# The last stores of a fused attention and mixture-of-experts kernel: an earlier signal, an earlier register read, one wait fewer

## The chip, the cores and the metric

The kernel runs on one core of a Trainium2 chip. A core has TensorE (PE in the profile), VectorE (DVE), ScalarE (ACT), GpSimd (POOL) and SyncE (SP), each with an instruction queue of its own, and 16 DMA engines. The metric is the device time of one execution in microseconds (us), the median over executions. The kernel before takes 640.18 us (median of 3: 639.88, 640.18, 641.45).

## The reference, cut to what matters

Three stages, all in float32, on 1152 tokens with 512 features:

```python
# 1. attention, 2 batches x 8 heads x 576 x 64, only the 32 largest scores of each row are kept
scores = q @ k.T / 8
mask = scores >= (32nd largest of the row)
attn = softmax(where(mask, scores, -1e9)); x = attn @ v
# 2. gated feed-forward: 512 -> 1536 -> 512
xn = x / sqrt(mean(x * x) + 1e-6) * rms_g
x = (silu(xn @ w_gate) * (xn @ w_val)) @ w_out
# 3. mixture of experts: 8 experts, each token goes to the one with the largest logit
e = argmax(x @ router, axis=1); gate = its softmax weight
slot = number of earlier tokens of that expert          # dropped if slot >= capacity = 288
out[token] = gate * (relu(x[token] @ w1[e]) @ w2[e])    # rows of dropped tokens are 0
```

## The kernel before, in words

Attention and the feed-forward run interleaved over 9 tiles of 128 tokens. At the end of each tile GpSimd scatters the token rows, each with its gate weight and its token number, to a DRAM tensor `dispatched_rows` ordered by expert. The change touches nothing there.

The last stage, the one at issue, is a chain over the experts 0 to 7. For each expert the kernel takes the first `MAIN` = 168 of its slots, as two halves (`j` = 0 and 1) of `SLOT` = 84 rows. SP loads the rows and the expert's weights, two experts ahead. For expert `e`:

- PE turns the rows (L842), multiplies by `w1` (`hidden`, L855) and by `w2` (`outputs`, L869) into a result that lies with features on partitions, and turns it back into rows (`turn_back`, L880): four transposes for half 0 into PSUM bank 6, then four for half 1 into bank 7. After the eighth it adds to the semaphore `y_done`.
- ACT scales half 0 by the gate weight (`rows_back` in the scalar block, L1234) and signals `y_act`; DVE does the same for half 1 (L1398) and signals `y_vec`. Both wait for `y_done`.
- GpSimd stores each half by an indirect DMA to the token's row of the output (`store`, L1588): first half 0, when `y_act` allows it, then half 1, when `y_vec` does. Each store adds 16 to its semaphore `stored[j][par]`, where `par` is the expert's parity.

`turn_back` of an expert stands behind `hidden` of the next one, so it is hidden there. For expert 7 nothing follows: its turn, scaling and stores are the end of the program.

If an expert has more than 168 tokens, the rest is done in a second pass. Whether that is so stands in the tile `most`, written by DVE beside expert 0 (L1384, semaphore `most_set`). PE, ACT, GpSimd and SP each read it into a register (`value_load`: L899, L1250, L1594, L410) and branch over the second pass. With this input no expert has so many.

At the end both GpSimd (L1606) and SP (L408) wait for all four `stored` semaphores; SP does so before it reads the count. Then the program's block closes (L94 in the trace): each engine executes a DRAIN, and all meet. In the trace PE, DVE, ACT and SP add to a semaphore with their DRAIN, GpSimd waits for these after its own, and then lets all go.

The order of each engine's instructions is as written in the code; no scheduler moves anything. Around the change the waits alone decide when something runs.

Of the kernel before, what the change touches and what calls it, by code (L numbers as in the profile page):

```python
# [61 lines left out]
def build(nc, q, k, v, w_gate, w_val, w_out, rms_g, r_gate, w1, w2, out, capacity):  # L62
    B, H, S, D = q.shape
    DM, FF = w_gate.shape
    E, _, F = w1.shape
    N = B * S
    NT = N // P
# [26 lines left out]
    with ctx:  # L94
# [3 lines left out]
        def sem(name):  # L98
            return ctx.enter_context(nc.semaphore(name))
# [47 lines left out]
        most = dest[:, 2:4]  # L147
# [44 lines left out]
        def gate_of(e, j):  # L192

            return meta[:, e, j, 0:1] if isinstance(e, int) else meta[:, bass.ds(e, 1), j, 0:1].rearrange("p a w -> p (a w)")
# [22 lines left out]
            "first_spots chosen out_full out_copied picked ranked_set lneg_set spot_base lexp_set gate_step row_ready seen_set dispatched last_dispatched most_set "  # L217

            "meta_in xs_in0 xs_in1 w1_a w1_b w2_a w2_b xt_done xt_act xt_vec h_done h_act h_vec "
            "yt_done yt_act yt_vec y_done y_act y_vec stored00 stored01 stored10 stored11 "  # L220

            "o_w o_x o_xt o_xtc o_h o_hc o_yt o_ytc o_y o_yc o_st o_free").split()
        s = {n: sem(n) for n in names}
# [8 lines left out]
        stored = [[s[f"stored{j}{par}"] for par in range(2)] for j in range(2)]  # L232
# [79 lines left out]
        def _(sp):  # L312
# [64 lines left out]
            def slots_in(e, par):  # L377
                sp.dma_start(xs[par], disp[bass.ds(e * CAP, MAIN), :].rearrange("(j p) w -> p j w", p=SLOT)).then_inc(xs_in[par], 16)
# [16 lines left out]
            def refill(e, par):  # L395

                sp.wait_ge(s["h_done"], e * 4 - 4)
                sp.dma_start(w1_s[par], w1[bass.ds(e, 1)].rearrange("a (c p) f -> p (a c) f", p=P)).then_inc(w1_in[par], 16)
                sp.wait_ge(s["yt_done"], e * 2 - 2)
                sp.dma_start(w2_s[par], w2[bass.ds(e, 1)].rearrange("a (c p) d -> p (a c) d", p=P)).then_inc(w2_in[par], 16)  # L400
                slots_in(e, par)

            with sp.Fori(1, E // 2) as i:
                refill(i * 2, 0)
                refill(i * 2 + 1, 1)
            for j in range(2):
                for par in range(2):
                    sp.wait_ge(stored[j][par], 8 * E)  # L408
            sp.wait_ge(s["most_set"], 1)
            over = sp.value_load(most[0:1, 0:1], min_val=0, max_val=N)  # L410
            with sp.If(over > MAIN):
                with sp.Fori(0, E) as e:

# [8 lines left out]
        def _(pe):  # L422
# [145 lines left out]
            def ffn_out(t, i):  # L568

                _, c0, c1 = OUT[i]  # L570
                for c in range(c0, c1):
                    if c % 4 == 0 or c == c0:
                        pe.wait_ge(s["t_free"], use[f"h{c // 4}", t] + 1)
                    last = mm(blk[0], hid[:, c * P:(c + 1) * P], wo_s[:, c, :], start=(c == 0), stop=(c == CF - 1))  # L574
                if i == len(OUT) - 1:
                    last.then_inc(s["out_full"], 1)
# [296 lines left out]
            def turn_back(e):  # L873
                pe.wait_ge(s["yt_act"], e + 2)
                pe.wait_ge(s["yt_vec"], e + 2)
                pe.wait_ge(s["y_act"], e + 1)
                pe.wait_ge(s["y_vec"], e + 1)
                for j in range(2):
                    for c in range(CD):
                        last = tr(ps[0:SLOT, 6 + j, c * P:(c + 1) * P], yT[:, c, j * SLOT:(j + 1) * SLOT], ident[:])  # L880
                last.then_inc(s["y_done"], 1)

# [4 lines left out]
            with pe.Fori(0, E // 2 - 1) as i:  # L888
                for par in (1, 0):
                    e = i * 2 + (1 if par else 2)  # L890
                    hidden(e, par)
                    turn_back(e - 1)
                    outputs(e, par)
            hidden(E - 1, 1)
            turn_back(E - 2)
            outputs(E - 1, 1, ahead=False)
            turn_back(E - 1)

            over = pe.value_load(most[0:1, 0:1], min_val=0, max_val=N)  # L899
            with pe.If(over > MAIN):  # L900
                with pe.Fori(0, E) as e:
                    pe.wait_ge(s["o_x"], e * 16 + 16)
                    pe.wait_ge(s["o_w"], e * 32 + 32)
                    for c in range(CD):
                        last = tr(ps[:, 0, c * REST:(c + 1) * REST], xs_all[0][0:REST, 0, c * P:(c + 1) * P], ident[0:REST, 0:REST])
                    last.then_inc(s["o_xt"], 1)
                    pe.wait_ge(s["o_xtc"], e + 1)
                    for f in range(C1):
                        for c in range(CD):
                            last = mm(ps[:, 2 + f // 4, (f % 4) * REST:(f % 4 + 1) * REST], w1_s[0][:, c, f * P:(f + 1) * P],  # L910
                                      xT[0][:, c, 0:REST], start=(c == 0), stop=(c == CD - 1))
                    last.then_inc(s["o_h"], 1)
                    pe.wait_ge(s["o_hc"], e + 1)
                    for d in range(CD):
                        for f in range(C1):
                            last = mm(ps[:, 4, d * REST:(d + 1) * REST], w2_s[0][:, f, d * P:(d + 1) * P],
                                      hT[:, f, 0:REST], start=(f == 0), stop=(f == C1 - 1))
                    last.then_inc(s["o_yt"], 1)
                    pe.wait_ge(s["o_ytc"], e + 1)
                    for c in range(CD):  # L920
                        last = tr(ps[0:REST, 6, c * P:(c + 1) * P], yT[:, c, 0:REST], ident[:])
# [4 lines left out]
        def _(act):  # L926
# [39 lines left out]
            def split_weights(m):  # L966

                raw, hi, _, half, cols = split_piece(m)
                act.wait_ge(s[("wg_in", "wv_in")[m // 2 % 2] + str(m // 4)], 16)
                for c in half:  # L970
                    copy(hi[:, c, cols], raw[:, c, cols]).then_inc(s["w_hi_set"], 1)
# [243 lines left out]
            def expert(e, par, back, ahead, later=True):  # L1215
                for n in (0, 2):
                    act.wait_ge(s["h_done"], e * 4 + n + 1)
                    nc.scalar.activation(hT[:, 2 * n:2 * n + 2, :], ps[:, 2, 0:2 * MAIN].rearrange("p (c n) -> p c n", c=2),
                                         ACT.Relu).then_inc(s["h_act"], 1)
                if back:  # L1220
                    rows_back(e - 1, 1 - par, later)
                act.wait_ge(s["yt_done"], e * 2 + 1)
                copy(yT[:, 0:2, :], ps[:, 4, 0:2 * MAIN].rearrange("p (c n) -> p c n", c=2)).then_inc(s["yt_act"], 1)
                if ahead:
                    slots(e + 1, 1 - par)

            def rows_back(e, par, later=True):
                act.wait_ge(s["y_done"], e + 1)

                if isinstance(e, int) and e == 0:  # L1230
                    act.wait_ge(s["meta_in"], 32)
                if later:
                    act.wait_ge(stored[0][par], (e - par) * 8)
                nc.scalar.activation(ys[par][:, 0, :], ps[0:SLOT, 6, :], ACT.Copy, scale=gate_of(e, 0)).then_inc(s["y_act"], 1)  # L1234
# [8 lines left out]
            with act.Fori(1, E // 2 - 1) as i:  # L1243
                expert(i * 2 + 1, 1, True, True)
                expert(i * 2 + 2, 0, True, True)
            expert(E - 1, 1, True, False)
            rows_back(E - 1, 1)

            act.wait_ge(s["most_set"], 1)
            over = act.value_load(most[0:1, 0:1], min_val=0, max_val=N)  # L1250
# [178 lines left out]
        def _(pool):  # L1429
# [164 lines left out]
            over = pool.value_load(most[0:1, 0:1], min_val=0, max_val=N)  # L1594
            with pool.If(over > MAIN):
                pool.sem_inc(s["o_free"], 1)
                for e in range(E):
# [3 lines left out]
                                          ys_all[0][0:REST, 0, :], None, bounds_check=N - 1, oob_is_err=False).then_inc(s["o_st"], 16)  # L1601
                    pool.wait_ge(s["o_st"], 16 * (e + 1))
                    pool.sem_inc(s["o_free"], 1)
            for j in range(2):
                for par in range(2):
                    pool.wait_ge(stored[j][par], 8 * E)  # L1606

# [18 lines left out]
```

## Time and profile before

| | |
|---|---|
| Median of 3 executions | 640.18 us (639.88 to 641.45) |
| The profiled execution's own time | 640.57 us |
| Its span, first to last instruction of the program | 638.8 us |
| Time around the span | 1.8 us |
| PE busy | 611.8 us, 96% of the span |
| DVE / ACT / POOL busy | 411.5 / 328.6 / 265.3 us |
| From the last expert's first transpose back (629.45 us) to the end of the span | 9.3 us |

The span is the time from the first to the last instruction of the program; in the profiled execution 1.8 us lie around it. A DMA's row tells how long the engine needs to issue it, and the data moves afterwards. At the very end nearly all engines show as idle, so shares of busy time say nothing; what is read there are the start times of the sequencers' instructions.

### The profile page before, as it was taken

Reading aid. Unit: us, or ns where it says so; the run is one execution under the profiler, and the core shown is the slowest. Engines: PE = TensorE matmul, PEld = TensorE weight load, DVE = VectorE, ACT = ScalarE, POOL = GpSimd, SP = SyncE. Lnnn points to the kernel's source line nnn. Section 1 sums busy time; section 2 is a strip of 40 time slices with the busy share of each in tenths; the row PEclk is TensorE's granted clock in tenths of the full one; section 3 lists DMA queues with packets and bytes.
Section 4 is the critical chain, followed back from the end, with each engine's and each line's share of the span. In section 5 each row is a group of like instructions: output and inputs, shape, how many; then the busy total and the mean of one; then the engine's idle time right before and its main releaser. Section 6 shows DMA issues by size and latency. Waiting matters only on the chain.

```text
span 638.8 us, 11148 instructions
## 1 busy us (share of the span) xinstructions
PE 611.8 (96%) x3935; PEld 470.0 (74%) x3935; DVE 411.5 (64%) x912; ACT 328.6 (51%) x713; POOL 265.3 (42%) x375
## 2 busy tenths in 40 slices
PE   7799989999999999999999999999999999999994
PEld 5466765875766766766766757757589999999994
DVE  5999999899898997998998998902011111011110
ACT  4777877766767766767756757653110110111100
POOL 1866875464365464553654555542310110011101
PEclk9899999999999999999999999999999999999998
DMA  9999800000000000000000000000696776766501
GB/s 239 214 360 337 244 14 0 16 20 2 17 18 1 18 18 2 16 18 2 18 18 2 1 18 2 9 9 1 211 384 185 263 270 208 279 216 235 174 2 39
DMA packets 55182, 65.45 MB, mean 102 GB/s; under 512 B 32282, under 2 KB 32282, under 8 KB 55132
## 3 DMA queue, kind: packets, MB, share of 16 engines
q1 hardware_dynamic: 53388, 60.05, 29.5%
q0 software_dynamic: 1744, 4.76, 2.0%
q8 instruction: 28, 0.46, 0.3%
q14 instruction: 22, 0.18, 0.1%
HBM read 52.89 MB, written 12.30 MB: 102 GB/s over the span
## 4 chain that ended last, share of the span: by engine, by line
PE 91%; ACT 3%; POOL 2%; issue 1%; DMA 1%; SPq 1%; DVE 0%; POOLq 0%; ACTq 0%
PE ps L574 14%; PE ps L869 12%; PE ps L855 11%; PE ps L526 7%; PE ps L533 7%; PE ps L527 7%; PE ps L507 7%; PE ps L480 6%; PE ps L491 6%; PE ps L465 4%; PE ps L589 2%; DMA w_loads<-in_moe_w_gate 1%; PE ps L702 1%; PE ps L880 1%; ACT pt L928 1%
## 5 line engine op out<-in xcount | busy, mean ns | idle before, releaser
L1563 POOL TENSOR_TENSOR s_ring<-s_ring,z_pair 128x576 f32<-128x576 f32 x72 | 100.7, 1420 | 68.9 <-ACT z_pair L1063 68.9
L1374 DVE MATCH_REPLACE8 w_top<-m,w_top 128x576 f32<-128x576 f32 x144 | 105.7, 741 | 0.0
L1368 DVE MAX8 m<-w_top 128x8 f32<-128x576 f32 x144 | 101.5, 745 | 0.0
L574 PE MATMUL ps<-wo_space,hid 128*128 128x512 f32 x216 | 100.7, 593 | 0.8 <-issue 0.8
L526 PE MATMUL ps<-w_parts,x_hi 128*128 128x512 f32 x196 | 81.7, 417 | 0.0
L527 PE MATMUL ps<-w_parts,x_hi 128*128 128x512 f32 x196 | 77.5, 395 | 0.0
L869 PE MATMUL ps<-arena,w_loads 128*128 128x168 f32 x512 | 75.8, 307 | 0.6 <-issue 0.6
L1588 POOL DMA_INDIRECT out_rows<-arena,s_ring x16 | 15.1, 941 | 147.0 <-DVE arena L1398 144.5
L855 PE MATMUL ps<-arena,w_loads 128*128 128x168 f32 x512 | 74.3, 306 | 0.6 <-ACT arena L928 0.6
L855 PEld LDWEIGHTS ps<-arena,w_loads 128*128 128x128 f32 x512 | 73.3, 190 | 0.9 <-ACT arena L928 0.9
L869 PEld LDWEIGHTS ps<-arena,w_loads 128*128 128x128 f32 x512 | 73.2, 190 | 0.8 <-issue 0.8
L1073 ACT ACTIVATE s_ring<-s_ring,nbias 128x576 f32<-128x576 f32 x72 | 55.5, 771 | 24.2 <-POOL s_ring L1563 24.1
L574 PEld LDWEIGHTS ps<-wo_space,hid 128*128 128x128 f32 x216 | 37.1, 190 | 31.2 <-issue 31.2
L1063 ACT ACTIVATE z_pair<-s_ring,nbias 128x576 f32<-128x576 f32 x72 | 51.7, 769 | 11.0 <-POOL nbias L1551 11.0
L928 ACT ACTIVATE pt<-ps 128x512 f32<-128x512 f32 (+1 forms) x108 | 48.8, 488 | 15.8 <-PE ps L491 15.8
L533 PE MATMUL ps<-w_parts,x_lo 128*128 128x512 f32 x196 | 56.8, 405 | 0.0
L1361 DVE MATCH_REPLACE8 w_top<-m,s_ring 128x576 f32<-128x576 f32 x72 | 53.2, 742 | 0.0
L1355 DVE MAX8 m<-s_ring 128x8 f32<-128x576 f32 x72 | 50.7, 744 | 3.3 <-ACT s_ring L928 3.1
L507 PE MATMUL ps<-pt,arena 128*64 128x128 f32 (+1 forms) x800 | 48.6, 271 | 4.2 <-ACT pt L928 4.2
L507 PEld LDWEIGHTS ps<-pt,arena 128*64 128x64 f32 x800 | 40.2, 139 | 15.8 <-issue 11.0
L1378 DVE MAX8 m<-w_top 128x8 f32<-128x576 f32 x72 | 50.8, 746 | 0.0
L928 ACT ACTIVATE s_ring<-ps 128x576 f32<-128x576 f32 x72 | 45.5, 647 | 9.6 <-PE ps L480 9.6
(143 smaller groups left out, 877.8 us busy)
## 6 DMA issues: line engine op xcount, KB each, us to landing
w_loads<-in_moe_w SPq DMA_DIRECT2D x16, 2048.0 KB, 8.9
dispatched_rows<-drow SPq DMA_DIRECT2D x18, 260.0 KB, 7.1
w_loads<-in_moe_w_gate SPq DMA_DIRECT2D x3, 1024.0 KB, 7.7
w_loads<-in_moe_w_val SPq DMA_DIRECT2D x3, 1024.0 KB, 9.9
wo_space<-in_moe_w_out SPq DMA_DIRECT2D x1, 3072.0 KB, 11.5
arena<-dispatched_rows SPq DMA_DIRECT2D x8, 341.2 KB
out_rows<-drow SPq DMA_DIRECT2D x9, 256.0 KB, 5.2
q_space<-in_q SPq DMA_DIRECT2D x8, 256.0 KB, 3.3
```

The costliest lines, as they stand in the source:

```text
L507: last = mm(oT_ps[a * D:(a + 1) * D, r0:r1], vs[b][:, j, 2 * hp + a, :], pt[:, at + r0:at + r1], start=(j == 0), stop=(j == KC - 1))
L526: mm(bank, x_hi[:, c * P:(c + 1) * P], w_hi[:, c, :], start=(c == 0), stop=False)
L527: mm(bank, x_hi[:, c * P:(c + 1) * P], w_lo[:, c, :], start=False, stop=False)
L533: last = mm(bank, x_lo[:, c * P:(c + 1) * P], w_hi[:, c, :], start=False, stop=(c == CD - 1))
L574: last = mm(blk[0], hid[:, c * P:(c + 1) * P], wo_s[:, c, :], start=(c == 0), stop=(c == CF - 1))
L855: last = mm(ps[:, 2 + n % 2, (f % 2) * MAIN:(f % 2 + 1) * MAIN], w1_s[par][:, c, f * P:(f + 1) * P], xT[par][:, c, :], start=(c == 0), sto ...
L869: last = mm(ps[:, 4 + n, (d % 2) * MAIN:(d % 2 + 1) * MAIN], w2_s[par][:, f, d * P:(d + 1) * P], hT[:, f, :], start=(f == 0), stop=(f == C ...
L928: return nc.scalar.activation(dst, src, ACT.Copy)
L1073: nc.scalar.activation(row, row, ACT.Exp, bias=nbias[:, 2 * (g % 2) + a:2 * (g % 2) + a + 1], accum_out=den[:, t % 2, h:h + 1]).then_inc(s ...
L1368: vec.max(m8[:, 2 * (n % 2) + a, i, :], w_top[:, a, :]).then_inc(s["top_step"], 1)
L1374: vec.match_replace(w_top[:, a, :], m8[:, 2 * (n % 2) + a, i, :], w_top[:, a, :], NEG).then_inc(s["top_step"], 1)
L1563: gp.tensor_tensor(row, row, z_pair[:, a, :], ALU.subtract).then_inc(s["lowered"], 1)
```

## The change

Three edits, all at the end of the program. `turn_back` adds to a new semaphore `y_half` after the fourth of the last expert's eight transposes, and ACT's last scaling waits for that in place of `y_done`. SP reads the overflow count before it waits for the stores rather than after. GpSimd no longer waits for the stores at its end.

```diff
-            "yt_done yt_act yt_vec y_done y_act y_vec stored00 stored01 stored10 stored11 "
+            "yt_done yt_act yt_vec y_half y_done y_act y_vec stored00 stored01 stored10 stored11 "
@@ SP
+            sp.wait_ge(s["most_set"], 1)
+            over = sp.value_load(most[0:1, 0:1], min_val=0, max_val=N)
+
             for j in range(2):
                 for par in range(2):
                     sp.wait_ge(stored[j][par], 8 * E)
-            sp.wait_ge(s["most_set"], 1)
-            over = sp.value_load(most[0:1, 0:1], min_val=0, max_val=N)
             with sp.If(over > MAIN):
@@ PE, turn_back
                     for c in range(CD):
                         last = tr(ps[0:SLOT, 6 + j, c * P:(c + 1) * P], yT[:, c, j * SLOT:(j + 1) * SLOT], ident[:])
+                    if j == 0 and isinstance(e, int) and e == E - 1:
+                        last.then_inc(s["y_half"], 1)
                 last.then_inc(s["y_done"], 1)
@@ ACT, rows_back
-                act.wait_ge(s["y_done"], e + 1)
+                if isinstance(e, int) and e == E - 1:
+                    act.wait_ge(s["y_half"], 1)
+                else:
+                    act.wait_ge(s["y_done"], e + 1)
@@ GpSimd, end of the block
-            for j in range(2):
-                for par in range(2):
-                    pool.wait_ge(stored[j][par], 8 * E)
```

The instructions of SP behind its last refill, in the kernel before. TENSOR_LOAD and the two ISA are the read of the count, COMPARE_AND_BRANCH is the jump over the second pass:

```order
L403 COMPARE_AND_BRANCH
L410 TENSOR_LOAD dest [waits stored11,stored10,most_set,stored01,stored00]
L410 ISA x2
L411 COMPARE_AND_BRANCH
```

and in the changed kernel:

```order
L403 COMPARE_AND_BRANCH
L407 TENSOR_LOAD dest [waits most_set]
L407 ISA x2
L412 COMPARE_AND_BRANCH [waits stored10,stored11,stored01,stored00]
```

The same three instructions now stand ahead of the wait, and only the branch is left behind it.

GpSimd's end in the kernel before, from the last store's issue over the count's read and the second pass (jumped over) to the block's end at L94:

```order
L1588 DMA out_rows<-arena,s_ring 1152x512 [waits y_vec,out_zero]
L1594 TENSOR_LOAD dest [waits most_set]
L1594 ISA x2
L1595 COMPARE_AND_BRANCH
L1600 DMA out_rows<-arena 1152x512 [waits o_yc,out_zero]
L1600 DMA out_rows<-arena 1152x512 [waits o_st,o_yc,out_zero] x7
L1595 UNCONDITIONAL_BRANCH [waits o_st]
L94 UNCONDITIONAL_BRANCH [waits stored10,stored11,stored01,stored00]
```

and in the changed kernel:

```order
L1594 DMA out_rows<-arena,s_ring 1152x512 [waits y_vec,out_zero]
L1600 TENSOR_LOAD dest [waits most_set]
L1600 ISA x2
L1601 COMPARE_AND_BRANCH
L1606 DMA out_rows<-arena 1152x512 [waits o_yc,out_zero]
L1606 DMA out_rows<-arena 1152x512 [waits o_st,o_yc,out_zero] x7
L1601 UNCONDITIONAL_BRANCH [waits o_st]
```

The wait at the end is gone and everything ahead of it stands as before.

## Rows read from the trace of the kernel before

**Rows 1.** Chain that ended last, from 619 us: start, duration (us), what.

```profile
618.91 0.76 PE ps L880 x7
619.67 9.13 PE ps L869 x64
...
629.45 1.06 PE ps L880 x8
630.51 0.02 issue
630.53 0.69 ACT arena L1234
631.23 0.02 issue
631.25 0.02 POOLq L1587
...
631.34 0.55 issue
631.89 0.02 POOLq L1587
...
632.12 0.92 POOL out_rows L1588
...
633.36 0.04 POOLq L1595
```

**Rows 2.** Timelines of ACT, DVE and POOL, from 628 us: start, duration, group, [idle before].

```profile
630.53 0.68 ACT L1234 ACTIVATE arena<-ps,s_ring 84x512 f32<-84x512 f32 x1 [5.80 <-PE ps L880]
...
630.53 0.75 DVE L1398 TENSOR_SCALAR arena<-ps,s_ring 84x512 f32<-84x512 f32 x1 [1.19 <-PE ps L880]
...
632.12 0.94 POOL L1588 DMA_INDIRECT out_rows<-arena,s_ring  x1 [8.65 <-DVE arena L1398]
633.36 0.93 POOL L1588 DMA_INDIRECT out_rows<-arena,s_ring  x1 [0.30 <-issue]
```

**Rows 3.** DMA issues, 631.5 to 640 us: count, median us from issue to landing.

```profile
out_rows<-arena,s_ring POOLq DMA_INDIRECT x2, 2.8
```

**Rows 4.** SP's queue, waits: us in total, times, longest.

```profile
SPq L408 <- DMA out_rows<-arena,s_ring: 45.0, 1, 45.0
```

**Rows 5.** Line L408, L410 and L411: count, duration min/median/max (ns), first and last start (us).

```profile
L408 SPq EVENT_SEMAPHORE  x1: 28/28/28, 636.2 to 636.2; - x1
...
L410 SPq TENSOR_LOAD <-dest x1: 484/484/484, 636.3 to 636.3; - x1
L410 SPq FUSED_REGOPS  x1: 183/183/183, 636.8 to 636.8; - x1
L410 SPq SEQ_ASSERT  x1: 26/26/26, 637.1 to 637.1; - x1
...
L411 SPq COMPARE_BRANCH  x1: 50/50/50, 637.2 to 637.2; - x1
```

**Rows 6.** Line L94, the block's end, columns as before.

```profile
L94 POOLq EVENT_SEMAPHORE  x2: 17/17/17, 638.6 to 638.7; - x2
...
L94 ACTq DRAIN  x1: 8/8/8, 631.5 to 631.5; - x1
...
L94 POOLq DRAIN  x1: 2122/2122/2122, 636.4 to 636.4; - x1
L94 SPq DRAIN  x1: 13/13/13, 637.3 to 637.3; - x1
```

**Rows 7.** Lines L1606 and L880: GpSimd's last waits, PE's turn back.

```profile
L1606 POOLq EVENT_SEMAPHORE  x2: 17/30/43, 633.5 to 636.2; - x2
...
L880 PE MATMUL ps<-ident,arena x64: 272/273/279, 500.2 to 630.2; 128*84 128x128 f32 x64
```

**Rows 8.** Line L1615, the block at the program's start.

```profile
L1615 POOLq DRAIN  x1: 174/174/174, 0.3 to 0.3; - x1
```

**Rows 9.** Lines L1384, L1588 and L900: writing the count; landing; PE's branch.

```profile
L1384 DVE CAST dest<-rt x1: 154/154/154, 481.2 to 481.2; 128x1 int32<-128x1 f32 x1
...
DMA to landing us min/median/max: 2.7/5.1/6.7
...
L900 PEldq COMPARE_BRANCH  x1: 348/348/348, 630.4 to 630.4; - x1
```

## The prediction

> **What bounds the kernel now.** The shares of the page (PE 96%) say that PE sets the time up to its last matmul, and the change takes nothing from there. So I read the end alone, in this order: the chain of waits from 619 us, the timelines of ACT, DVE and POOL, the time to landing, and then, line by line, the sequencers' instructions behind the last store. [rows 1] shows PE's eight transposes from 629.45, ACT's scaling right behind at 630.53, GpSimd released at 631.25, its first store issued at 632.12 and the second at 633.36 [rows 2]. A store lands 2.8 us after its issue [rows 3], so the second has landed at 633.36 + 2.8 = 636.2, and there SP's wait of 45.0 us ends [rows 4, 5]. The chain as printed stops at the second issue; what fills 636.2 to 638.8 must be read from the block's end. There two arrivals compete: SP reads the count and comes to its DRAIN at 637.3 [rows 5, 6]; GpSimd comes to its DRAIN at 636.4, and that takes 2.122 us, to 638.5 [rows 6]. The others have long arrived (ACT at 631.5). So GpSimd's DRAIN ends last, and between its end at 636.4 + 2.12 = 638.55 and the end at 638.8 lies about 0.23 us of meeting. The reader is to see that SP's arrival has 638.55 - 637.34 = 1.2 us to spare.
>
> **Part 1, the half signalled alone.** Eight transposes take 1.04 to 1.06 us [rows 1], one lasts 0.273 [rows 7], so they start (1.04 - 0.27) / 7 = 0.11 us apart, and the fourth ends 4 x 0.11 = 0.44 us ahead of the eighth. ACT has been idle for 5.8 us until then [rows 2], and its other wait, for the store of expert 5, is long over. Its scaling starts at 630.09 and signals at 630.79. GpSimd's first wait ends 0.44 earlier, its sequencer comes to the second wait at 631.89 - 0.44 = 631.45, and DVE, whose start is unchanged, ends at 630.53 + 0.75 = 631.28 [rows 2]: just in time, with 0.17 us left. Two issues stand 633.36 - 632.12 = 1.24 us apart whatever DVE does. So the second store is issued at 632.92 and lands at 636.16 - 0.44 = 635.72. The added signal sits on a transpose that is issued anyway. Bounds: 0 if ACT can't use it, and 0.44 + 0.17 = 0.61 us at most, where DVE becomes what GpSimd waits for. I take 0.44.
>
> **Part 2, the count read early.** TENSOR_LOAD 484, FUSED_REGOPS 183 and SEQ_ASSERT 26 ns are 0.69 us, and with four gaps of 0.03 to 0.04 as those in [rows 1] 0.83 us [rows 5]. They move into SP's idle 45.0 us, which begin at 636.2 - 45.0 = 591.2, and the count has been there since 481.2 [rows 9], so they cost nothing there, and nothing is queued behind them but the wait. Behind the wait stay the branch and the DRAIN: SP arrives 0.83 earlier, by itself. Alone this is worth 0, since GpSimd arrives 1.2 us later than SP.
>
> **Part 3, GpSimd's wait dropped.** Its last waits begin at 633.5 [rows 7], right behind the branch at 633.36 [rows 1]; with part 1 its DRAIN can start at 633.1. It must outlast the second issue, 632.92 + 0.93 = 633.85. The trace shows no DRAIN with a store in flight. From below: 0.174 us, that of the start of the program [rows 8], which would end it at 634.0. From above: its 2.12 us counted anew from the landing at 635.72, so to 637.84. Between them: 2.12 us counted from the last issue's end, 633.85 + 2.12 = 635.97. I take the last, because in the profiled run the 2.12 us pass when all stores have landed and the engine has been idle since 634.3 [rows 2, 6]: nothing of this program is left to wait for, so it is work of the DRAIN's own, which can be done beside the stores.
>
> The Trainium skill, page "VectorE: DVE Perf Modes", section "The DRAIN you can't avoid", says that the DRAINs that frame a kernel are about 12 ns and constant on all engines. SP's 13 ns and ACT's 8 ns [rows 6] agree, GpSimd's 2122 ns don't, and the measurement decides. [...]
>
> **The sum.** SP arrives at 637.34 - 0.83 - 0.44 = 636.07, GpSimd at 635.97: SP is now last, by 0.1 us, and the end comes at 636.07 + 0.23 = 636.30. That is 638.78 - 636.30 = 2.48 us less. The parts do not add up one by one: part 3 alone would leave SP last at 637.34 (1.2 us gained), part 2 on top gives 0.8 more, part 1 the last 0.44. The profiled execution took 640.57, which becomes 638.09; it lies 0.39 above the median of the runs, so as a median 640.18 - 2.48 = 637.7 us, 0.39% less.
>
> **Rivals.**
> A. The DRAIN's 2.12 us begin only when the stores have landed. For it: in the one case that the trace has, they did. Against it: in that case GpSimd itself was kept from starting it earlier. GpSimd arrives at 637.84, the end is 638.07, 0.7 us gained: 639.5 us. Nearly the whole gain of parts 2 and 3 would be gone, since SP's earlier arrival is then again of no use.
> B. The DRAIN is partly hidden: part of its steps are done beside the stores and part wait for them, or each goes slower while descriptors and data move. Half of it behind the landing gives 635.72 + 1.06 = 636.78, the end at 637.0, 1.8 us gained: 638.4 us; three quarters give 638.9.
> C. Part 1 doesn't do what it says: ACT does not start before the eighth transpose, or the sequencer's 0.55 us before its next wait [rows 1] do not move along. Then landing stays at 636.16, SP arrives at 636.51, 2.04 us gained: 638.1 us. Against it: ACT starts 0.02 us behind the transposes' end and GpSimd 0.02 us behind ACT's, so each hangs on the one before.
> D. The other side. GpSimd both writes the stores' descriptors and executes the DRAIN, which now begins during the second store. If it holds that store up, the landing is late. The nearest row is the slowest landing of a store, 6.7 us [rows 9] against 2.8; those had weight loads beside them, so it is an upper bound. Landing at 632.92 + 6.7 = 639.6, SP 0.35 us (637.34 - 0.83 - 636.16) and the meeting 0.23 behind it: 640.2, 1.4 us slower, 641.6 us. It decides the sign from a landing time of 2.8 + 2.48 = 5.3 us on. Against it: the second issue's descriptors are written within its 0.93 us, before which the DRAIN can hardly be served.
>
> The Trainium skill, page "Runtime: NRT & Kernel Launch", section "Instruction fetch mechanics", says that a taken branch to code outside the loaded pages must wait until it is fetched. SP's branch is now the only instruction of the kernel's own behind the landing. Its 50 ns [rows 5] show no such wait; the 348 ns of PE's [rows 9] may. By the rule SP would arrive up to 0.3 us later; by the row nothing changes, and I leave it at nothing.
>
> **How the numbers follow.** Forecast 60%, A 15%, B 13%, C 8%, D 4%. About 0.3% or 1.9 us is what a measurement of this kernel can tell from no change. Forecast (2.48) is over it, but by 0.6 us only, and medians of few runs move by some 0.3 us (the fastest of the three runs before lies 0.3 below the median): I count 53 of its 60 as faster. C (2.04) lies on the bound: 4 of 8. B (1.3 to 1.8) 2 of 13, A none. That makes faster 0.59, same 0.37, slower 0.04. The likeliest case's own range is 637.2 to 638.2. To hold 8 in 10 the range must also reach C, B and A: 637.1 to 639.6. The upper end is A's; the lower is the forecast less twice the 0.3 us by which medians move.
>
> **What would show it.** In the changed kernel's trace: ACT's last scaling starts before the eighth transpose ends and some 0.44 us before DVE's; the issues remain 1.24 us apart; SP's TENSOR_LOAD is at about 591 us, and behind its wait at 635.7 only branch and DRAIN (to 636.1); GpSimd's DRAIN starts at about 633.1 and ends by 636.0, and lasts up to 2.9 us, for it includes the second issue. If it ends at 637.8, A is right; in between, B; if the second store lands over 2.8 us after its issue, D is at work. The prediction is wrong if GpSimd still arrives last by more than 0.2 us.

## The result, and the profile after

The changed kernel takes 638.43 us (median of 7 executions, 638.01 to 639.84) against 640.18 (median of 7, 639.63 to 641.47): 1.75 us less, a ratio of 0.9973 with a 95% interval of 0.9962 to 0.9983. The whole interval lies below 1, so the gain is clear of the noise, though at 0.27% it is slightly under the 0.3% that the prediction took as the least that such a measurement can tell. The forecast was 637.7 in a range of 637.1 to 639.6: right way, inside the range, 0.7 us too low.

The profiled execution of the changed kernel took 639.84 us, the slowest of its seven, and its span is 638.0. Compare ends, not spans: the last expert's first transpose starts at 630.45 here and at 629.45 before, and in the executions below it starts anywhere from 628.2 to 630.5, also in two of the same kernel (630.45 here, 628.73 in e11_after); the last section says what goes with it. From that start to the end of the span it takes 7.59 us instead of 9.33. The difference, 1.74 us, is the gain as the two traces show it. Below, "the tail" is this stretch.

The timeline of the changed kernel from 628 us, start, duration, group and [idle before], answers to [rows 1, 2]:

```profile
630.45 1.04 PE L881 MATMUL ps<-ident,arena 128*84 128x128 f32 x8 [0.65 <-issue]
631.09 0.68 ACT L1240 ACTIVATE arena<-ps,s_ring 84x512 f32<-84x512 f32 x1 [5.36 <-PE ps L881]
631.53 0.75 DVE L1404 TENSOR_SCALAR arena<-ps,s_ring 84x512 f32<-84x512 f32 x1 [1.18 <-PE ps L881]
632.68 0.94 POOL L1594 DMA_INDIRECT out_rows<-arena,s_ring  x1 [8.21 <-DVE arena L1404]
633.92 0.94 POOL L1594 DMA_INDIRECT out_rows<-arena,s_ring  x1 [0.30 <-issue]
```

ACT now starts 0.44 us ahead of DVE, while the transposes still run to 631.49; before, both started at 630.53. The two issues are 1.24 us apart as before. The landing takes 2.8 us as in [rows 3].

The lines L407 (the count's read), L411 and L412 of SP, and L94, the block's end, of the changed kernel, with count, duration min/median/max in ns, first and last start in us; they answer to [rows 5, 6]:

```profile
L407 SPq TENSOR_LOAD <-dest x1: 477/477/477, 592.2 to 592.2; - x1
...
L411 SPq EVENT_SEMAPHORE  x2: 17/22/28, 626.3 to 636.7; - x2
...
L412 SPq COMPARE_BRANCH  x1: 50/50/50, 636.8 to 636.8; - x1
...
L94 POOLq EVENT_SEMAPHORE  x2: 17/17/17, 637.8 to 637.9; - x2
...
L94 POOLq DRAIN  x1: 3721/3721/3721, 634.1 to 634.1; - x1
L94 SPq DRAIN  x1: 13/13/13, 637.0 to 637.0; - x1
```

SP reads the count at 592.2, deep in its idle time, its wait ends at 636.7 with the landing, and it is through at 637.0. GpSimd's DRAIN starts at 634.1, beside the second store's issue, and lasts 3.72 us, to 637.8. So it is still GpSimd that arrives last, 1.08 us behind the landing, where it had been 2.39 us.

### The profile page after: what moved, and what is told of

Its sections match the earlier page's. It is cut to its first block, busy times and chain, and to the rows that moved or that the text cites. A ratio compares the mean times of both kernels' runs of the same rounds, so it can differ in the third digit from the quotient of the medians.

```text
span 638.0 us, 11145 instructions
## 1 busy us (share of the span) xinstructions
PE 613.7 (96%) x3935; PEld 471.0 (74%) x3935; DVE 411.4 (64%) x912; ACT 328.7 (52%) x713; POOL 265.9 (42%) x375
## 4 chain that ended last, share of the span: by engine, by line
PE 92%; ACT 3%; POOL 2%; issue 1%; DVE 0%; POOLq 0%; ACTq 0%
PE ps L575 14%; PE ps L870 12%; PE ps L856 11%; PE ps L527 8%; PE ps L534 7%; PE ps L528 7%; PE ps L508 7%; PE ps L481 7%; PE ps L492 6%; PE ps L466 5%; PE ps L590 2%; PE ps L703 1%; PE ps L881 1%; PE ps L559 1%; ACT pt L931 1%
## 5 line engine op out<-in xcount | busy, mean ns | idle before, releaser
L575 PEld LDWEIGHTS ps<-wo_space,hid 128*128 128x128 f32 x216 | 37.1, 190 | 31.2 <-issue 31.2
L1384 DVE MAX8 m<-w_top 128x8 f32<-128x576 f32 x72 | 50.8, 747 | 0.0
```

## The experiments

Each kernel is one of the two with the edit shown. What its trace, of one execution each, says is collected here. "Landing" is the last increment of the stores' semaphores, "DRAIN" the one at the end of the program, "since" how many DMAs GpSimd has issued between the previous DRAIN and this one; all times in us. e3 and e6 to e10 were run once each, so their times say little and their traces are what counts.

| kernel | parts | since | tail | DRAIN lasts | DRAIN ends behind landing | SP arrives behind landing |
|---|---|---|---|---|---|---|
| before | none | 25 | 9.33 | 2.12 | 2.39 | 1.18 |
| e1_half | 1 | 25 | 8.90 | 2.12 | 2.39 | 1.18 |
| e3_half_early | 1, 2 | 25 | 8.89 | 2.12 | 2.39 | 0.28 |
| e2_nowait | 3 | 25 | 8.11 | 3.72 | 1.08 | 1.18 |
| e7_nowait_early | 2, 3 | 25 | 8.03 | 3.73 | 1.08 | 0.28 |
| after | 1, 2, 3 | 25 | 7.59 | 3.72 | 1.08 | 0.28 |
| e11_after (after again) | 1, 2, 3 | 25 | 7.61 | 3.74 | 1.08 | 0.28 |
| e8_drain_first | 1, 2, 3 | 16 | 7.23 | 3.36 | 0.70 | 0.28 |
| e4_drain6 | 1, 2, 3 | 2 | 6.78 | 2.76 | 0.12 | 0.28 |
| e12_drain6 (e4 again) | 1, 2, 3 | 2 | 6.80 | 2.77 | 0.12 | 0.28 |
| e9_drain6_late_read | 1, 3 | 2 | 7.67 | 2.75 | 0.12 | 1.18 |
| e10_before_drain_first | none | 16 | 8.57 | 1.36 | 1.63 | 1.18 |
| e5_before_drain6 | none | 2 | 8.13 | 0.22 | 0.48 | 1.18 |
| e6_drain_all | none | 2 | 8.12 | 0.21 | 0.48 | 1.18 |

The tail repeats well (7.59 and 7.61, 6.78 and 6.80) where whole executions scatter by more than 1 us, so the verdicts on the parts rest on it. In all 14 the second store lands 2.8 us after its issue.

**The parts one by one.** First part 1 alone:

```diff
 # e1_half: the kernel before, with
+                    if j == 0 and isinstance(e, int) and e == E - 1:
+                        last.then_inc(s["y_half"], 1)
...
-                act.wait_ge(s["y_done"], e + 1)
+                if isinstance(e, int) and e == E - 1:
+                    act.wait_ge(s["y_half"], 1)
+                else:
+                    act.wait_ge(s["y_done"], e + 1)
```

> Part 1 alone: the last expert's first half is signalled after four transposes, both other edits undone. All theories: from the start of the last expert's transposes to the end of the span 9.33 us before, so 9.33 - 0.44 = 8.89 here, with GpSimd's DRAIN still 2.1 us long behind the landing. As a median 0.4 us less than before, too little for the timing to tell. If ACT or GpSimd's sequencer can't use the signal, 9.33.

Tail 8.90, so 0.43 less: as expected. Its ratio to before, 0.9988 (0.9979 to 0.9997), agrees with it. The next has part 3 alone:

```diff
 # e2_nowait: the kernel before, without
-            for j in range(2):
-                for par in range(2):
-                    pool.wait_ge(stored[j][par], 8 * E)
```

> Part 3 alone: GpSimd's wait for the stores dropped, both other edits undone. Theory 'partly hidden' (the DRAIN ends 1.1 us behind the landing of the last store, whatever went before): GpSimd arrives at about the same time as SP, which still reads the count behind the landing (1.18 us behind it): from the transposes to the end 9.33 - 1.2 = 8.1 us. Rival 'own work' (2.12 us counted from the end of the last issue): the same 8.1 us, but the DRAIN ends 0.3 us behind the landing and SP is last by 0.9 us. The two differ in where GpSimd's DRAIN ends.

Tail 8.11, ratio 0.9974 (0.9964 to 0.9983). The two theories differed in where the DRAIN ends. These are the rows of L94 and of L408, SP's wait, of this kernel:

```profile
L94 POOLq DRAIN  x1: 3723/3723/3723, 634.0 to 634.0; - x1
L94 SPq DRAIN  x1: 13/13/13, 637.8 to 637.8; - x1
...
L408 SPq EVENT_SEMAPHORE  x1: 28/28/28, 636.7 to 636.7; - x1
```

Landing at 636.64, DRAIN from 634.0 to 637.7: 1.08 us behind the landing, not 0.3. My "own work" theory, on which the forecast stood, falls; "partly hidden" holds. Then the remaining pairs:

```diff
 # e3_half_early: the changed kernel, GpSimd's wait kept
+            for j in range(2):
+                for par in range(2):
+                    pool.wait_ge(stored[j][par], 8 * E)
 # e7_nowait_early: the changed kernel, y_half gone, ACT waiting for y_done again
...
-                    if j == 0 and isinstance(e, int) and e == E - 1:
-                        last.then_inc(s["y_half"], 1)
...
-                if isinstance(e, int) and e == E - 1:
-                    act.wait_ge(s["y_half"], 1)
-                else:
-                    act.wait_ge(s["y_done"], e + 1)
+                act.wait_ge(s["y_done"], e + 1)
```

> Parts 1 and 2 without part 3: GpSimd's wait for the stores stays. All theories: GpSimd's DRAIN of 2.12 us behind the landing sets the end, the early read is worth nothing, and from the transposes to the end it is the 8.9 us of part 1 alone. SP arrives 0.35 us behind the landing.

> Parts 2 and 3 without part 1. GpSimd's DRAIN ends 1.08 us behind the landing as in the changed kernel and is last; SP arrives 0.35 us behind it. From the transposes to the end 7.59 + 0.44 = 8.03 us. That is only 0.1 less than with part 3 alone (8.11), so part 2 is worth 0.1 us in this kernel and not 0.83.

Tails 8.89 and 8.03, as expected. So the early read is worth nothing while GpSimd waits and drains (8.90 to 8.89), and 0.08 us once it drains beside the stores (8.11 to 8.03). Of the three edits it does the least in this kernel. In e3 the timing of the one execution, 641.22 us, lies above before's median though its tail is 0.43 shorter; its last transposes began at 630.54. One execution says nothing on a tenth of a per cent here.

**What the DRAIN does.** In the kernel before nothing is in flight when it starts, and yet it takes 2.12 us; GpSimd's DRAIN at the program's start took 0.17 [rows 8]. One explanation is that it looks at each DMA that GpSimd has issued since its last DRAIN: nine scatters of rows to the experts and sixteen stores. GpSimd idles 8 us before the last expert's stores, so a further DRAIN can be put there:

```diff
 # e4_drain6: the changed kernel; e5_before_drain6: the kernel before; both with
             for e in range(E):
                 store(e, e % 2)
+                if e in (6,):
+                    gp.drain()
```

> The changed kernel with one more DRAIN on GpSimd, behind the stores of expert 6, where it idles 8.6 us. Theory 'list' (a DRAIN looks at each DMA that GpSimd has issued since its last DRAIN: 9 scatters and 16 stores, 2.12 us / 25 = 0.085 us each): the added DRAIN takes those 23 and ends by 628, hidden; the last one has two DMAs and ends 0.1 to 0.3 us behind the last landing, SP is last, from the transposes to the end 6.9 us against 7.59 of the changed kernel, 0.8 us less as a median (637.6). Rival 'fixed' (a DRAIN behind DMAs costs the same however many there are): the last one ends 1.1 us behind the landing as in the changed kernel, 7.6 us, same median, 638.4.

> The kernel before with one more DRAIN on GpSimd, behind the stores of expert 6. GpSimd's wait for the stores stays, so the last DRAIN starts when all has landed. Theory 'list': it lasts about 2 x 0.085 us plus the 0.17 of an idle DRAIN or less, in place of 2.12; SP is last, and from the transposes to the end 9.33 - 1.2 = 8.1 us. Rival 'fixed': 2.1 us and 9.33 as before.

The rows of L94 of e5_before_drain6, and behind them the added DRAIN:

```profile
L94 POOLq DRAIN  x1: 220/220/220, 635.7 to 635.7; - x1
L94 SPq DRAIN  x1: 13/13/13, 636.6 to 636.6; - x1
```

```profile
L1594 POOLq DRAIN  x1: 4534/4534/4534, 620.9 to 620.9; - x1
```

With the same code behind it, the last DRAIN falls from 2122 to 220 ns because another ran 15 us earlier. SP is now last, and the tail is 8.13, though not a line of the change is in. The executions agree: median 639.04 us (10) against 640.20 (30), a ratio of 0.9977 (0.9966 to 0.9988). In e4_drain6:

```profile
L94 POOLq EVENT_SEMAPHORE  x2: 17/17/17, 636.5 to 636.6; - x2
...
L94 POOLq DRAIN  x1: 2761/2761/2761, 633.6 to 633.6; - x1
L94 SPq DRAIN  x1: 13/13/13, 636.5 to 636.5; - x1
```

The DRAIN ends 0.12 behind the landing, SP 0.28 behind it, and the tail is 6.78. "List" holds, "fixed" falls. The median, 638.32 us, did not show the 0.8 us that were expected (637.6); the two kernels are timed side by side further down. The next two tell what is counted, and how much of it the stores can hide:

```diff
 # e8_drain_first: the changed kernel; e10_before_drain_first: the kernel before; both with
+            gp.drain()
             for e in range(E):
                 store(e, e % 2)
```

> The kernel before with one more DRAIN on GpSimd ahead of the first store; the wait for the stores stays, so the last DRAIN finds all landed. It tells whether DMAs are counted or rows. By DMAs (2.122 us for 25, 0.220 for 2: 0.083 each): 0.22 + 14 x 0.083 = 1.38 us for the 16 stores. By rows (9 scatters of 128 rows and 16 stores of 84, 2496 rows in all, 168 in the last two stores, 0.82 ns a row): 1.18 us. If neither, and only a DRAIN near the end shortens it: 2.12.

It lasts 1.36 us against 1.38 by DMAs and 1.18 by rows. By packets (in the trace 80 for a scatter and 64 for a store) it would be 1.28. DMAs fit best:

```profile
L94 POOLq DRAIN  x1: 1363/1363/1363, 636.7 to 636.7; - x1
```

> The changed kernel with one more DRAIN on GpSimd ahead of the first store, so that the last DRAIN has the 16 stores on its list and not the 9 scatters. It starts while the second store is in flight. Theory 'two sweeps' (the list is gone through twice, 0.042 us each time per DMA, and the second time behind the last landing: 1.08 us with 25 DMAs, 0.11 with 2): it ends 0.11 + 14 x 0.042 = 0.70 us behind the landing. Rival 'one slowed sweep' (0.083 us per DMA when idle, 0.14 with a store in flight, so 13 of 25 were done at the landing): 13 of 16 are done, and it ends 0.3 us behind the landing. From the transposes to the end: 7.2 us by the first, 6.8 by the second.

```profile
L94 POOLq DRAIN  x1: 3356/3356/3356, 633.2 to 633.2; - x1
L94 SPq DRAIN  x1: 13/13/13, 636.1 to 636.1; - x1
```

It ends 0.70 us behind the landing at 635.84, as "two sweeps" said to the hundredth; "one slowed sweep" said 0.3 and falls. The tail is 7.23. And a DRAIN after each expert:

```diff
 # e6_drain_all: the kernel before, with
+                if e in (0, 1, 2, 3, 4, 5, 6):
+                    gp.drain()
```

> The kernel before with a DRAIN on GpSimd behind the stores of each of the experts 0 to 6. By the list theory the first (11 DMAs) ends 0.11 + 9 x 0.042 = 0.49 us behind its landing, each later one (2 DMAs) 0.1 us, and the last, with all landed, lasts 0.22 us as with a single added DRAIN. Span as with that one, since GpSimd idles in between. If what a DRAIN costs grows with all DMAs of the program, the later ones end up to 1.1 us behind their landing.

The first added one, with 11 DMAs, ends 0.50 us behind its landing, the other six, with 2 each, 0.12, and the last lasts 0.21:

```profile
L94 POOLq DRAIN  x1: 210/210/210, 637.5 to 637.5; - x1
```

```profile
L1594 POOLq DRAIN  x7: 3627/6207/7509, 504.4 to 622.8; - x7
```

So an added DRAIN is long because it waits for its stores: 6.1 to 7.5 us for the first five, which have weight loads beside them, and 3.6 for the last two, behind the last weight load. GpSimd idles there anyway, and the tail is that of e5_before_drain6 (8.12 and 8.13). Together: with all landed, 2.12, 1.36 and 0.22 us for 25, 16 and 2 DMAs, 0.083 a DMA; with the last in flight, 1.08, 0.70, 0.50 and 0.12 behind the landing for 25, 16, 11 and 2, 0.042 a DMA. The added DRAINs of the other kernels give two more points on the second line: with 9 DMAs (the scatters, e8 and e10) one ended 0.42 us behind the last scatter's landing, with 23 (e4, e5, e9, e12) 0.99. Half of the time per DMA can pass while DMAs fly, half comes behind the last landing.

**Part 2 again, where nothing covers it.**

```diff
 # e9_drain6_late_read: e4_drain6, with SP's read behind its wait as before
-            sp.wait_ge(s["most_set"], 1)
-            over = sp.value_load(most[0:1, 0:1], min_val=0, max_val=N)
-
             for j in range(2):
                 for par in range(2):
                     sp.wait_ge(stored[j][par], 8 * E)
+            sp.wait_ge(s["most_set"], 1)
+            over = sp.value_load(most[0:1, 0:1], min_val=0, max_val=N)
```

> The changed kernel with the added DRAIN behind the stores of expert 6, but with SP reading the count behind its wait, as in the kernel before. With GpSimd's DRAIN short, SP alone sets the end and part 2 is worth its full 0.83 us: from the transposes to the end 6.78 + 0.83 = 7.61 us. Rival: the read is hidden anyway, 6.8 us.

Tail 7.67 against 6.78: the same edit that is worth 0.08 us beside part 3 is worth 0.88 here, 0.05 more than expected. SP's DRAIN comes 0.90 us later behind the landing; the 0.83 left out that SP's wait for `most_set` moves with the read. It stands at L409 of the kernel before, and from it to the read's start it takes 0.07 us:

```profile
L409 SPq EVENT_SEMAPHORE  x1: 28/28/28, 636.2 to 636.2; - x1
```

**A version that beats both.** The changed kernel and the one with the added DRAIN, on one chip:

> The changed kernel itself, on the same chip as the next. From the transposes to the end 7.6 us, 1.7 us less than before as a median (ratio 0.9973).

> The changed kernel with the added DRAIN behind the stores of expert 6, against the changed kernel on the same chip. The list theory: 6.8 us from the transposes to the end, so 0.8 us less than the changed kernel as a median and 2.5 us (0.4%) less than before, ratio 0.9960. Rival: in executions without a profile's detail the DRAIN costs less than the trace says, and both kernels have one median.

Medians 638.84 us (11 executions) and 637.89 (5) against 640.50 for the kernel before; ratios to before 0.9974 (0.9964 to 0.9983) and 0.9962 (0.9948 to 0.9976). In the earlier measurement e4_drain6 had 638.32 and 0.9965 (0.9954 to 0.9976). Both kernels beat the one before. That the added DRAIN beats the changed kernel is shown by the tails, twice 0.81 us shorter; by the times alone the intervals overlap. All executions of both chips together point the same way (638.60 over 18, 638.06 over 13).

## Why the prediction was right, and where it was not

- **What bounds the end.** Right. GpSimd's DRAIN was last, SP had 1.2 us to spare, and from the last arrival to the end it takes 0.21 to 0.24 us in every trace (0.23 by forecast).
- **Part 1**, forecast 0.44: measured 0.43 (before to e1) and 0.44 (e7 to after). DVE ended 0.17 us ahead of the wait that needs it, as forecast. Rival C falls.
- **Part 2**, forecast to bring SP forward by 0.83, alone worth 0: SP came 0.90 earlier (1.18 to 0.28 behind the landing), for the wait at L409 went with the read. It was not run quite alone; beside part 1, with GpSimd's wait kept, it was worth 0.01. In the sum it was given 0.8; it brought 0.08, because GpSimd stayed last.
- **Part 3**, the step that failed: "it is work of the DRAIN's own, which can be done beside the stores". The DRAIN's time does go with what GpSimd has issued, but only half of it can pass there. Forecast was a DRAIN from 633.85 + 2.12 = 635.97, which is 0.25 behind the landing; it ended 1.08 behind. By the sign that the prediction set for itself, "GpSimd still arrives last by more than 0.2 us", its mechanism was wrong: GpSimd is last by 0.80 us (1.08 - 0.28). Alone the part was worth 1.22 us, as forecast (1.2), but that was luck of the pair: SP was 1.18 behind the landing there, and so covered the DRAIN's 1.08.
- **The sum**, 2.48 forecast and 1.74 measured in the tail: the last arrival was forecast 0.35 us behind the landing (SP) and came 1.08 behind it (GpSimd), which is 0.73 of the 0.74. The added DRAIN takes GpSimd out of the way, and its tail of 6.78 us is close to what the forecast had for the changed kernel (9.33 - 2.48 = 6.85). The median, 638.43, missed the likeliest case's own range (637.2 to 638.2); it lies in the stated one because that was drawn wide enough to reach B and A.
- **Rivals.** It was B. "Half of it behind the landing" (1.06 us, 638.4 us) met both the trace (1.08) and the median (638.43), and had 13%. A asked for 2.12 behind the landing. D did not show: the landing took 2.8 us in every kernel. Nor did the wait for instructions that was weighed for SP's branch: it took 50 ns before and after. The 12 ns by the Trainium skill's page "VectorE: DVE Perf Modes", section "The DRAIN you can't avoid", which it gives for the DRAINs of the runtime's own preamble and postamble, are near those of SP (13 ns) and ACT (8 ns) at the block's end. They do not hold there for DVE, whose DRAIN starts beside its last scaling and takes 786 ns, or for GpSimd after DMAs: 0.21 to 3.74 us, by what it has issued and what is in flight.

The evidence was at hand for a better weighing. A DRAIN of 0.17 us without DMAs and 2.12 with 25 suggested that its time hangs on DMAs. What hangs on a DMA may need that DMA to be over, so B deserved more than 13% against the 60% of the forecast.

## What to carry to other kernels

When GpSimd has issued DMAs and arrives last at a program's end, look at its DRAIN: it can be shortened from outside, by a DRAIN in earlier idle time. Here that cost nothing that the tails show; where the engine has no idle time of some microseconds it was not tried. And when two engines race to a meeting, price each edit against the other engine's arrival: the same early read was worth 0.01, 0.08 and 0.88 us, depending on what stood beside it. For effects of a tenth of a per cent, compare the stretch from a fixed instruction to the end, which repeated to 0.02 us in the two kernels traced twice, and not whole executions.

## What the runs showed of the hardware

- GpSimd's DRAIN costs 0.083 us for each DMA that GpSimd has issued since its previous DRAIN, besides some 0.05, even when all have landed (2.12, 1.36 and 0.22 us for 25, 16 and 2). Rows, and bytes, which go with them, don't fit (1.36 for 16 stores, 1.18 by rows). The DRAIN of 0.17 us at the program's start, with no DMA, ended 0.05 us behind the last of four MEMSETs.
- Started with a DMA in flight, it ends 0.041 to 0.042 us per DMA, plus some 0.04, behind the last landing (0.12, 0.42, 0.50, 0.70, 0.99 and 1.08 us for 2, 9, 11, 16, 23 and 25). That the list is gone through twice, the second time behind the landing, is how I read these two slopes; what the engine does inside was not seen.
- A DRAIN alone makes GpSimd wait for its stores without a semaphore wait: in e6_drain_all each ended 0.12 us or more behind its landing, never ahead of it.
- Where the last transposes begin moves between 628.2 and 630.5 us from execution to execution, not with the edits: the changed kernel has 630.45 in one and 628.73 in another. These 1.7 us are there by 75 us of the span and stay to the end: 1.2 are there by 27 us, another 1.2 come up to 35 us, and 0.7 are lost again. The middle part goes with the clock that TensorE was granted: half (1.2 GHz) for 6.8 us in the one, from 27.8 to 34.6 us, and for 3.4 us in the other, from 27.8 to 31.2. The stretch 31.5 to 34.5 us of both, first `after`, then `e11_after`, with us, busy time of each engine, granted clock, DMA share and GB/s:

```profile
31.50:34.50 3.00, 3.00 (x6) 1.20 (x7) 3.00 (x8) 2.10 (x4) 2.37 (x3) 0.50 1.02 376
31.50:34.50 3.00, 3.00 (x18) 1.80 (x17) 3.00 (x9) 2.17 (x5) 3.00 (x3) 1.00 1.01 368
```

In the four traces with the full clock back by 31.5 us (e1, e5, e7, e11) the last transposes begin at 628.2 to 629.0, in the four where it comes back at 34.4 or later (e9, e3, after, e6) at 630.4 to 630.5. No run here changes the clock by itself, so a cause is not shown, and where the other parts come from is open.
